# Reordering the first loads of a fused attention and expert kernel: values 0 asked for behind queries and keys 1, queries and keys 4 ahead of values 3

## What is computed

```python
for c in range(nc):                                  # chunks of 32 queries, 8 heads of 64
    k_full = concat(mem_k, k[c_start-16 : c_end+8])  # 8 memory keys and up to 56 own ones
    scores = scale * q_c @ k_full.T
    a = exp(scores - max); a = a / (sum(a) + 1e-9)
    out[c] = a @ v_full
h = x @ w_in                                         # dense layer, 512 -> 2048 -> 512
x = (h * sigmoid(1.702 * h)) @ w_out
e = argmax(x @ w_gate)                               # eight experts, at most 384 tokens each
out[i] = gate_w[i] * (relu(x[i] @ w1[e]) @ w2[e])
```

## Time and profile before

| | |
|---|---|
| median of 3 runs | 507.27 us (507.15 to 507.57) |
| the profiled execution's own time | 506.39 us |
| its span, first to last instruction | 504.7 us |
| mean granted TensorE clock | 0.995 |
| TensorE busy | 487.7 us, 97% |
| VectorE, ScalarE, GpSimd busy | 310.9, 219.7, 163.1 us |
| moved by DMA | 76.93 MB, 152 GB/s on average |

### The profile page before, as it was taken

How to read it: one execution, slowest core, us unless ns; L and a number is a source line. 1 busy time by engine, 2 the same in 40 slices (tenths; PEclk the granted TensorE clock), 3 DMA queues, 4 the chain that set the end, 5 groups by cost and what they waited for, 6 DMA issues and landing times.

```text
span 504.7 us, 9477 instructions
## 1 busy us (share of the span) xinstructions
PE 487.7 (97%) x3529; PEld 403.1 (80%) x3529; DVE 310.9 (62%) x677; ACT 219.7 (44%) x384; POOL 163.1 (32%) x190
## 2 busy tenths in 40 slices
PE   7899999999999999999999999999999999999992
PEld 4788888888888887888888778798888878888882
DVE  5576555454267775225777777855578878638760
ACT  3655545433231222123212556324367858847620
POOL 3411110000000000300000037064157999999942
PEclk9999999999999999999999999999999999999997
DMA  7999821498500000201233336125796978956000
GB/s 254 285 274 274 266 72 44 139 329 245 166 1 1 0 2 0 85 0 43 84 96 113 94 134 190 44 87 149 240 361 225 347 275 307 349 188 250 24 28 33
DMA packets 26719, 76.93 MB, mean 152 GB/s; under 512 B 5279, under 2 KB 5279, under 8 KB 26400
## 3 DMA queue, kind: packets, MB, share of 16 engines
q1 hardware_dynamic: 22656, 69.77, 42.1%
q0 software_dynamic: 4000, 6.32, 3.5%
HBM read 62.92 MB, written 19.96 MB: 164 GB/s over the span
## 4 chain that ended last, share of the span: by engine, by line
PE 83%; DVE 5%; DMA 4%; issue 4%; ACT 2%; DVEq 1%; another core or an unknown queue 0%; POOL 0%; SPq 0%; ACTq 0%; POOLq 0%
PE bank L1362 10%; PE bank L1363 10%; PE bank L1364 10%; PE bank L1406 9%; PE bank L1408 9%; PE bank L1407 8%; PE bank L1375 7%; DMA tile_in<-attention_tiles 3%; PE bank L1643 3%; PE bank L1377 3%; PE bank L1645 3%; PE bank L1647 3%; PE bank L1646 3%; PE bank L1353 2%; PE bank L1318 2%
## 5 line engine op out<-in xcount | busy, mean ns | idle before, releaser
L391 POOL TENSOR_TENSOR w_lo<-raw,w_hi 128x256 fp32r<-128x256 f32 x104 | 91.7, 916 | 9.5 <-ACT w_hi L375 9.5
L665 ACT ACTIVATE g<-bank 128x512 f32<-128x512 f32 x48 | 28.6, 596 | 134.1 <-PE bank L1364 134.1
L578 POOL DMA_INDIRECT dispatched_rows<-rows,slot_idx x12 | 12.8, 1070 | 219.4 <-DVE slot_idx L1075 216.6
L375 ACT ACTIVATE w_hi<-raw 128x1024 fp32r<-128x1024 f32 x80 | 82.0, 1050 | 2.3 <-DMA raw<-dense_units 2.0
L391 DVE TENSOR_TENSOR w_lo<-raw,w_hi 128x1024 fp32r<-128x1024 f32 (+1 forms) x60 | 69.8, 1173 | 19.1 <-ACT w_hi L375 18.3
L1406 PE MATMUL bank<-w_hi,g_hi 128*128 128x512 f32 x192 | 77.3, 402 | 0.0
L1362 PE MATMUL bank<-x_hi,w_hi 128*128 128x512 f32 x192 | 77.1, 402 | 0.0
L1408 PE MATMUL bank<-w_hi,g_lo 128*128 128x512 f32 x192 | 75.8, 395 | 0.0
L1407 PE MATMUL bank<-w_lo,g_hi 128*128 128x512 f32 x192 | 75.8, 395 | 0.0
L1363 PE MATMUL bank<-x_lo,w_hi 128*128 128x512 f32 x192 | 75.7, 394 | 0.0
L1364 PE MATMUL bank<-x_hi,w_lo 128*128 128x512 f32 x192 | 75.6, 394 | 0.0
(11 more groups left out here) (154 smaller groups left out, 816.2 us busy)
## 6 DMA issues: line engine op xcount, KB each, us to landing
raw<-expert_units SPq DMA_DIRECT2D x64, 512.0 KB, 6.4
raw<-dense_units SPq DMA_DIRECT2D x16, 512.0 KB, 5.1
tile_in<-attention_tiles SPq DMA_DIRECT2D x12, 592.0 KB, 5.2
dispatched_rows<-empty SPq DMA_DIRECT2D x26, 257.0 KB, 8.1
slot_rows<-dispatched_rows SPq DMA_DIRECT2D x26, 257.0 KB
tile_in<-attention_tiles SPq DMA_DIRECT2D x12, 384.0 KB, 5.7
gate_rows<-gate_rows SPq DMA_DIRECT2D x2, 1024.0 KB, 5.1
out<-rows,e_token POOLq DMA_INDIRECT x16, 3.6
```

The costliest lines, as they stand in the source:

```text
L375: act.activation(w_hi[u % RING][:, :], raw[u % RING][:, :], ACT.Copy).then_inc(s_whi, 1)
L391: last = engine.tensor_tensor(w_lo[u % RING][:, part], raw[u % RING][:, part], w_hi[u % RING][:, part].bitcast(F32), ALU.subtract)
```

## The change

It touches the written order of the sync engine's first loads alone. V0 is asked for when QK1 has landed, no longer when QK2 has. U0 is asked for right behind V1, ahead of the wait for V0. QK4 changes places with V3 and their waits with them. U1 stays behind the wait for V2. QK5 waits for QK4 and no longer for V3, and the first load of the loop behind it, U2, for V3 and no longer for QK4.

```diff
             load_queries_keys(3)
-            landed_queries_keys(2)
+            landed_queries_keys(1)
             load_values(0)
             landed_queries_keys(3)
             load_values(1)
+            load_unit(0)
             landed_values(0)
-            load_unit(0)
             load_values(2)
             landed_values(1)
+            load_queries_keys(FIRST)
+            landed_unit(0)
             load_values(3)
-            landed_unit(0)
-            load_queries_keys(FIRST)
             landed_values(2)
             load_unit(1)
+            landed_queries_keys(FIRST)
+            load_queries_keys(FIRST + 1)
             landed_values(3)
-            load_queries_keys(FIRST + 1)
-            landed_queries_keys(FIRST)
             unit = 2
```

## The result

The change made the kernel slower: 509.61 us against 507.38 us, medians of 22 runs each, ratio 1.004 with a 95% interval of 1.0026 to 1.0055. That is 2.0 us by the ratio, twice what can be told from no change, and outside the range given. The kernel was run again later with fresh runs of before beside it: 508.97 against 507.06, ratio 1.0033 (1.0015 to 1.0051). So there are two profiles of the change; the first took 509.57 us with a span of 507.8, near the median; the second 507.80 with 506.1, a short one among its 12 runs (507.41 to 510.96).

What follows compares the result with a forecast made beforehand. TensorE, 83% of the chain, bounds the kernel; only the dense layer's start could move. V3 at 20.0 plus 2.55 puts it at 22.55 instead of 22.97: 0.4 us off the median 507.27, forecast 506.85 us, range 505.9 to 508.05.

Steps and rivals of the forecast that it cites:

- the fifth: V3's load: asked for at U0's landing, 15.5, lands at 20.0 instead of 19.70 us; dense start 2.55 us after it.
- the second rival: V3 lands so late that the dense start moves back: 0.8 to 1.7 us slower, 508.05 to 508.95 us; chance 0.14.
- step 2: U0's load: asked for at 10.2 instead of 12.39, lands at 15.5 us, 0.9 us earlier; alone it gives nothing.
- The third step: V2's load: asked for at V0's landing, follows U0, lands at 16.8 us; needed at 18.1, so no longer matters.
- no term comes from it: Granted clock: reads 1.00 in both early stretches of before, so it adds nothing to the forecast.
- The first step: V0's load: lands at 11.2, 1.2 us earlier; TensorE gains 0.61 us, passed down the engines' chain without loss.
- the fourth step: QK4's load: lands at 18.7 instead of 21.90, scores(4) stop waiting for it; worth at most 0.65 us.
- whole cover: V3 lands by 19.2, only the engines' chain is left: dense start 21.75, 1.2 us gained, 506.05 us; chance 0.15.

Runs made afterwards that it cites:

- the third edit: Part of the change: QK4 asked for ahead of V3, with the waits that go with it.
- the swap alone: Kernel before with only QK4 put ahead of V3 (QK4 asked for at V1's landing, V3 at U0's): 509.57 against 507.20 us, ratio 1.0047.
- the change with no late block: The change plus two sync engine waits, V0 also for half of scores(1), U0 for half of scores(3): 509.17 against 507.31 us, ratio 1.0035.
- the fill: Nine unread matmuls between values(2) and values(3), added to the swap alone: 508.41 against 507.06 us, ratio 1.0026; added to the change: 509.42 against 507.25, ratio 1.0042.
- U0 alone: Kernel before with only U0 moved, asked for right behind V1, ahead of the wait for V0: 506.64 against 507.31 us, ratio 0.999.
- all but V0: The change with V0 waiting for QK2 again, as before: 508.44 against 507.20 us, ratio 1.0034.
- V3 behind QK4: The swap alone with V3 asked for right behind QK4 at V1's landing, no longer at U0's: 510.39 against 507.06 us, ratio 1.0052.
- U0 and V3 early: U0 alone with V3 also asked for right behind V2 at V0's landing: 506.77 against 507.06 us, ratio 0.9996.
- gate: An added sync engine wait that holds a load back: V0 until half of scores(1), U0 until half of scores(3).
- The first edit: Part of the change: V0 asked for when QK1 has landed; put alone into the kernel before: 508.35 against 507.31 us, ratio 1.001.

## Why the prediction was wrong

**The step that failed is the fifth, V3's landing.** It put V3 at 20.0, and the sum drew from that a gain of 0.4 us. V3 landed at 22.6 and 21.6 in the two profiles of the change, and at 21.3 to 23.2 in the seven other runs with the third edit. Every run with the third edit is slower with an interval above 1, among them the swap alone (1.0047) and the change with no late block (1.0035); none of the runs without it is. That is the second rival, mechanism and place; it had a chance of 0.14 and was priced at 0.8 to 1.7 us, without stops and clock.

The other part of the fifth step, 2.55 us from V3's landing to the dense start, held: 21.63 + 2.55 = 24.18 in the second profile, where 24.26 was measured. In the first it gives 22.59 + 2.55 = 25.14 of the 26.22. There no matmul waited for V3, because the stop in values(1) and the half clock had made TensorE later still; without them V3 alone would have cost 2.2 of the 3.25 us. So that profile has two causes, each enough for most of its loss, and only the runs apart from it tell them apart.

Three sizes went into the 20.0, and all were too small:

- U0 was to land at 15.5. Its last share came at 16.7 and 16.9. In the second profile 15 of the 16 shares had landed by 14.9 and the last came at 16.89, just after the instruction block (15.70 to 16.77) had passed. What a wait sees is the slowest of 16.
- Transfers were costed by bytes, 1.3 us for values. By first shares U0, V2, QK4 and V3 came at 15.7, 17.4, 19.0 and 20.6 in the first profile and at 14.5, 16.3, 18.4 and 20.4 in the swap alone: 1.6 to 2 us each, 393 kB or 606; in the second profile of the change 1.4 and 1.7, and 2.6 for V3, which was asked for only at 16.90. The 1.64 us each that step 2 found in before was the better rule, and I did not use it: from 15.5 it gives 20.4, no gain at all, and from U0's real 16.7 it gives 21.6. The third step erred the same way: V2 was to land at 16.8 and landed at 18.2 in both profiles.
- The last share of V3 came 2.0 and 1.7 us behind its first in the two profiles, against 1.0 in before. In the first profile 15 shares of V3 had landed by 20.92 and the last came at 22.59, the moment at which a block ended (21.59 + 1.00).

**That "no term comes from it", from the clock, was wrong.** Of 109 runs of before (those of the experiments) 16 had a mean granted clock of 0.992 or less, of 34 of the change 15. Where it fell, the run was 1.7 to 1.8 us longer (before 507.1 against 508.8 on average; the change 508.7 against 510.5). Taken all as the clock's, that is 0.3 x 1.8 = 0.5 us of the mean loss of 2.1. This is an estimate and rather a bound from above, since the runs with a low clock may be those with the longer waits. In single profiles the half clock cost 1.0 us (values(2) and (3) in the change) to 1.45 (values(3) and scores(4) in the swap alone), and the fill took 1.0 of the swap's 2.4 away. How the rest of the whole change divides between V3 and late blocks stays open: they overlap, since a stop in values(1) delays values(2) and hides part of the wait for V3 or all of it.

**The first step failed too, at "It runs down the engines' chain without loss".** V0 came earlier (11.8 and 10.8 instead of 12.38), but the 0.61 us were never earned: TensorE stopped in scores(3) for its instructions, with V0 ahead of them, and values(0) began at 13.22 and 12.99 instead of 12.42. The slip of QK2 that the step took as nil was nil (7.84 and 7.98 against 8.09); QK3's was not, 10.99 in the first profile against 9.80. The row of before had the trace of it: scores(3) took 1.45 us where the other scores take 1.10, and I read past it.

And the 0.61 us stood in one profile only. In the six runs that left V0 where it was (U0 alone, all but V0, the swap alone, with the fill, V3 behind QK4, U0 and V3 early), V0 landed at 11.2 to 11.7 and values(0) began at 11.58 to 11.98 without a wait for it. In the six profiles in which it was asked for at QK1's landing with no gate ahead, at 5.9 to 6.1 us instead of 7.4 to 8.1, it landed at 10.8 to 13.3. The first edit set out to remove a wait that one of seven profiles had.

**Right:** QK4 stopped being what scores(4) waits for; V3 was the next late load, and values(3) waited for it (second profile, 0.94 us; in the first the stop covered the wait); U1, QK5 and U2 did no harm; the shift of the dense start was carried to the end (3.25 us and 3.1, 1.3 and 1.4). U0 alone gained 0.65 us in its profile, the most that the fourth step gave QK4's landing. The "whole cover" rival was the farthest off: the Trainium skill ("DMA: Bandwidth & Descriptors", "Anatomy of one DMA") gives the fit that it names, 2.9 us for V3, for transfers issued by GpSimd, while these are the sync engine's, and V3 took 5.9 and 4.7 us.

## What to carry to other kernels

A load that is moved ahead of another costs that other one its whole transfer, by first shares mostly 1.6 to 2 us here, for 384 and 592 KB alike; before taking a load off the critical place, work out the landing of the one that it overtakes with the time per transfer that full stretches of the same profile show, and add the spread between first and last share. Instructions are data too: a deep queue of loads delays the instruction blocks of an engine that runs through many small instructions, and gaps inside a group of like instructions with "issue" behind them are the sign. A wait of some tenths of a us in one profile can be that execution's alone: look for it in a second profile of the same kernel before building an edit on it. Waits of 1 to 2 us on TensorE cost more than themselves when the granted clock falls behind them.

## What the runs showed of the hardware

- TensorE's instruction blocks (16 KB, 0.93 to 1.9 us each on the DMA engines before 30 us) started only when data asked for before them were landing: 4.8 us after TensorE had gone on from the last one in the first profile of the change, 1.5 in before. When a block is asked for is not in the trace. The Trainium skill ("DMA: Bandwidth & Descriptors", "Queues, rings and completion order") has an engine take turns between queues packet by packet; if the request comes where it is inferred above, a block here did not get ahead of the two or three transfers queued by then, and the measurement decides.
- In three places where a block passed, one of the 16 shares of a transfer beside it landed 1.2 to 2.0 us after the other 15, and so the whole transfer (QK3 and V3 in the first profile, U0 in the second, each at the block's end). That they are on the same DMA engine was read from the times that coincide, and not tried by itself. It is not the only case: QK4 in the first profile had 15 shares by 19.46 and the last at 21.41, with no block on the queue from 18.44 to 21.59.
- After TensorE had been idle for 1.6 to 2.6 us ahead of values(3), the granted clock fell to 0.50 in the gap or up to 1.7 us behind it in all four profiles in which nothing filled it; with a fill and the same landing it stayed at 1.00. After 0.94 us, in the second profile of the change, it stayed too, and so it did for 5.4 us behind the stop of 2.51 us in "all but V0". An idle stretch of 2 us does not always bring the clock down.
- A wait that is already met took TensorE about 50 ns an instruction: 60 of them 2.9 us.
